# Attention and two dense layers on one core: order of the attention output copy, of the first dense slot, of the last keys' bank and of one store

## The reference

```python
# 1. attention, batch 4, 8 heads, 576 positions, head dimension 64
scores = (1/sqrt(64)) * q @ k.T + bias          # bias: a small net of |i-j| and i, per head
attn = exp(scores - rowmax) / (rowsum + 1e-9)
x = concat_heads(attn @ v)                      # 2304 tokens x 512
# 2. first dense layer, 512 -> 2048 -> 512
h = x @ w_in
y = (h - tanh(h)) @ w_out
# 3. second dense layer, 512 -> 1536 -> 512
g = y @ w_gate
out = (g * sigmoid(g) * (y @ w_val)) @ w_out2
```

## Time and profile before

| | us |
|---|---|
| median of 3 runs | 1259.72 |
| lowest and highest of them | 1258.40, 1260.73 |
| the profiled execution, its own time | 1260.17 |
| its span, first to last instruction | 1258.4 |
| PE busy | 1182.5 (94%) |
| DVE, ACT, POOL busy | 606.4, 574.2, 520.7 |
| bias table | to about 75 |
| plain heads and edge slot | about 75 to 138 |
| unit 0 with its eight large slots | 138 to 259 |
| units 1 and 2, large slots | 259 to 491 |
| units 3 and 4, short slots | 491 to 728 |
| rest of the first layer, second dense layer | to the end |

### The profile page before, as it was taken

How to read it: one execution, slowest core, us unless ns; L and a number is a source line. 1 busy time by engine, 2 the same in 40 slices (tenths; PEclk the granted TensorE clock), 3 DMA queues, 4 the chain that set the end, 5 groups by cost and what they waited for, 6 DMA issues and landing times.

```text
span 1258.4 us, 20260 instructions
## 1 busy us (share of the span) xinstructions
PE 1182.5 (94%) x7320; PEld 1082.7 (86%) x7320; DVE 606.4 (48%) x1377; ACT 574.2 (46%) x1163; POOL 520.7 (41%) x584
## 2 busy tenths in 40 slices
PE   5778799999999998999999999999999999999998
PEld 2345588889888988999899999999999999999998
DVE  8966677665566555666666643521211212112111
ACT  6977566655555555555555554521212222122212
POOL 2036577655555554877777722111111111111111
PEclk9999899999999999999999999999999999999999
DMA  5887464343434332544445343300000000000000
GB/s 172 260 264 222 129 190 143 110 128 104 115 108 128 110 99 81 156 133 139 138 142 137 111 157 126 126 26 1 27 26 26 26 22 30 1 26 1 26 1 26
DMA packets 80067, 125.46 MB, mean 100 GB/s; under 512 B 19424, under 2 KB 42976, under 8 KB 79968
## 3 DMA queue, kind: packets, MB, share of 16 engines
q1 hardware_dynamic: 79968, 124.17, 32.9%
HBM read 104.07 MB, written 20.05 MB: 99 GB/s over the span
## 4 chain that ended last, share of the span: by engine, by line
PE 76%; DVE 11%; issue 5%; ACT 5%; DMA 1%; SPq 1%; DVEq 0%; ACTq 0%
PE ps_s L1535 12%; PE ps_y L1546 12%; PE ps_h L1423 11%; PE ps_y L1442 11%; PE ps_h L1535 6%; PE ps_pt L1535 6%; PE ps_s L1343 5%; PE ps_pt L1362 5%; PE ps_pt L1396 3%; DVE feat L1058 3%; DVE prob L1091 2%; DVE g_b L1124 1%; PE ps_pt L1423 1%; ACT tanh_b L810 1%; DVE xy_stage L1132 1%
## 5 line engine op out<-in xcount | busy, mean ns | idle before, releaser
L723 POOL TENSOR_TENSOR fr<-tanh_b,fr 128x384 fp32r<-128x384 f32 x72 | 73.1, 1016 | 378.0 <-ACT fr L988 378.0
L1442 PE MATMUL ps_y<-fr,wbuf 128*128 128x384 f32 x1152 | 225.7, 336 | 0.0
L666 POOL TENSOR_SCALAR prob<-prob,rowinv 128x576 f32<-128x576 f32 (+1 forms) x160 | 122.4, 765 | 210.8 <-DVE rowinv L1102 195.0
L1423 PE MATMUL ps_h<-fr,wbuf 128*128 128x384 f32 x1056 | 206.6, 340 | 0.5 <-DVE g_b L1124 0.4
L1442 PEld LDWEIGHTS ps_y<-fr,wbuf 128*128 128x128 f32 x1152 | 198.9, 188 | 0.0
L1423 PEld LDWEIGHTS ps_h<-fr,wbuf 128*128 128x128 f32 x1056 | 181.9, 189 | 1.4 <-DVE g_b L1124 0.9
L785 ACT ACTIVATE prob<-prob,negmax 128x576 f32<-128x576 f32 (+1 forms) x160 | 124.0, 775 | 119.1 <-DVE negmax L1091 118.6
L1546 PE MATMUL ps_y<-wbuf,fr 128*128 128x512 f32 x648 | 161.1, 393 | 0.0
L671 POOL TENSOR_TENSOR fr<-g_b,fr 128x384 fp32r<-128x384 f32 x96 | 96.7, 1007 | 126.5 <-ACT fr L816 126.4
L1546 PEld LDWEIGHTS ps_y<-wbuf,fr 128*128 128x128 f32 x648 | 120.5, 188 | 22.1
L1362 PE MATMUL ps_pt<-ident,prob 128*128 128x128 f32 (+1 forms) x640 | 87.7, 264 | 40.4 <-DVE xy_stage L1132 26.3
(11 more groups left out here) (128 smaller groups left out, 1952.5 us busy)
## 6 DMA issues: line engine op xcount, KB each, us to landing
biasb<-bias_scratch SPq DMA_DIRECT2D x128, 216.0 KB, 2.7
raw<-k_t SPq DMA_DIRECT2D x59, 288.0 KB, 3.0
bias_scratch<-w_raw SPq DMA_DIRECT2D x72, 144.0 KB, 3.2
biasb<-bias_scratch SPq DMA_DIRECT2D x64, 144.0 KB, 2.9
w_raw<-w_chunks SPq DMA_DIRECT2D x16, 512.0 KB, 5.6
prob<-w_chunks SPq DMA_DIRECT2D x8, 768.0 KB, 4.2
raw<-v_p SPq DMA_DIRECT2D x32, 160.0 KB, 2.3
biasb<-bias_scratch SPq DMA_DIRECT2D x64, 72.0 KB, 2.6
```

Source lines behind the costliest of these rows:

```text
L666: eng.tensor_scalar(row, row, rowinv[0:hd.rows, tile % PR:tile % PR + 1], 1.0, ALU.mult, ALU.mult).then_inc(p_norm, 1)
L1423: mm = eng.matmul(hidden_bank(u, c)[:, 0:TOK], w[:, cols], x[:, d, :], start=d == 0 and i == 0, stop=d == KC - 1 and i == 2)
L1442: mm = eng.matmul(ps_y[:, d, 0:TOK], w[:, cols], g[c % 2], start=c == 0 and i == 0, stop=c == C1 - 1 and i == 2)
```

## The change

- **Large slots.** On ACT `o_part` of head v comes ahead of `tanh` of the slot's second chunk and its `g_high`; on DVE `x_out` comes ahead of that chunk's `gated`. It was the other way round.
- **First dense slot** (unit 0, chunks 0 and 1). `tanh` and `gated` of chunk 0 are the first work of ACT and DVE; PE's `gaps` become `[4, 2, 0]`, so chunk 1's hidden pieces come after tile 0 and two model pieces after tile 1. `inverse` of tile 1 of head 8 moves into the edge slot. In the edge slot ACT computes both exponentials before `o_part`, and DVE scores both tiles before `x_out`.
- **Last keys of plain heads** go to bank `ps_h` (tile 1's) instead of `ps_pt` (tile 0's). The wait for their copy moves from tile 0's transposes to tile 1's, the transposes of the last keys wait for tile 1's copy, and DVE's `pt_copy_end` moves ahead of `inverse` of tile 1. The first hidden piece of all waits for that bank too.
- **Short slots.** In a unit's last slot ACT's `x_high` comes before `o_part`, and DVE's `x_low` of the last quarter comes after `inverse`.
- **SP** issues the first quarter of `store_y` before the load of q instead of after it; in units with large heads the load of q comes later anyway, so nothing changes there.

```diff
@@ SP, loop over heads
                 following = HEADS[n + 2:n + 3]
+                if hd.unit > 1 and n == FIRST_OF[hd.unit] + 1:
+                    store_y(hd.unit - 2, 0)
                 for nxt in following:
                     if not ended(hd):
                         load_q(nxt)
                 for t in range(hd.nt):
-                    if t == 0 and hd.unit > 1 and n == FIRST_OF[hd.unit] + 1:
-                        store_y(hd.unit - 2, 0)
@@ ACT, edge
                 o_part(HEADS[v.n - 1], moe)
                 exp_tile(q, 0)
+                exp_tile(q, 1)
                 o_part(v, moe)
                 q_high(p, moe)
-                exp_tile(q, 1)
@@ ACT, short
                 g_high(u, c)
+                if late(moe):
+                    x_high(u + 1)
                 o_part(v, moe)
                 if q is not None:
                     exp_tile(q, 1)
-                if late(moe):
-                    x_high(u + 1)
@@ ACT, slot
+                if v.n == H:
+                    tanh(*moe[0])
                 pt_high(v, 0, moe)
...
                 exp_tile(q, 0)
-                if not first:
+                if not first and v.n > H:
                     tanh(*moe[0])
...
                 for t in range(2, q.nt):
                     exp_tile(q, t)
+                o_part(v, moe)
                 tanh(*moe[1])
                 g_high(*moe[1])
-                o_part(v, moe)
@@ DVE, pt_copy_end
-                eng.tensor_copy(plain_end(hd), ps_pt[64:P, 0:TOK]).then_inc(v_pt, 1)
+                eng.tensor_copy(plain_end(hd), ps_h[64:P, 0:TOK]).then_inc(v_pt, 1)
@@ DVE, alone
+                    if t == q.nt - 1 and v is not None:
+                        pt_copy_end(v)
                     if t > 0:
                         inverse(q, t - 1)
-                if v is not None:
-                    pt_copy_end(v)
@@ DVE, edge
                 score(q, 0, moe)
+                score(q, 1, moe)
+                inverse(q, 0)
                 x_out(v, moe)
                 x_high_last(0)
                 x_low(0, 1)
-                inverse(q, 0)
-                score(q, 1, moe)
+                inverse(q, 1)
+                score(q, 2, moe)
                 q_low(p, moe)
-                score(q, 2, moe)
@@ DVE, short
                     x_high_last(u + 1)
-                    x_low(u + 1, 1)
                 if q is not None:
                     inverse(q, 1)
                 if late(moe):
+                    x_low(u + 1, 1)
                     x_low(u + 1, 0)
@@ DVE, slot
+                if v.n == H:
+                    gated(*moe[0])
                 pt_low(v, 0, moe)
                 if v.n == H:
-                    inverse(v, 1)
                     inverse(v, 2)
...
-                if not first:
+                if not first and v.n > H:
                     gated(*moe[0])
...
+                x_out(v, moe)
                 gated(*moe[1])
-                x_out(v, moe)
@@ PE, transposed (plain heads)
-                    if t == 0:
+                    if t == 1:
                         eng.wait_ge(v_pt, splits(last, 0) + 1)
@@ PE, transposed_end
-                    eng.wait_ge(a_pt, copies(hd, 0) + 1)
+                    eng.wait_ge(a_pt, copies(hd, 1) + 1)
                 for t in range(hd.nt):
-                    mm = eng.transpose(ps_pt[:, tile_cols(hd, t)], prob[:, (hd.tile0 + t) % PR, S - P:S], ident[:, :])
+                    mm = eng.transpose((ps_pt if moe else ps_h)[:, tile_cols(hd, t)], prob[:, (hd.tile0 + t) % PR, S - P:S], ident[:, :])
@@ PE, hidden_pieces
+                        if (u, c) == (0, 0):
+                            eng.wait_ge(v_pt, splits(HEADS[H], 0))
@@ PE, slot
                 if moe[0] == (0, 0):
                     layer_work(4)
-                    gaps = [0, 0, 2]
+                    gaps = [4, 2, 0]
```

## The result

| | before | changed |
|---|---|---|
| median, us | 1260.09 (4 runs, 1258.40 to 1260.73) | 1241.99 (4 runs, 1241.34 to 1242.51) |
| the profiled execution, its span | 1260.17, 1258.4 | 1242.15, 1240.3 |
| PE busy | 1182.5 | 1179.8 |

The ratio is 0.9858, with a 95% interval of 0.9841 to 0.9875: the changed kernel is faster by 1.4%, 18.1 us. I had said 1248.5 (1242 to 1255); the median lies at the lower end of that range. So the direction is right and the size is a third too small.

The account below looks back on a forecast made before the run. PE sets the pace in units 1 and 2, stopping once per slot for `x_out`; ACT and DVE bound about half of unit 0's slots. Terms -12.6+2.6+2.1+1.5-1.6-3.3 = -11.3 us gave 1248.5 (1242 to 1255).

Parts of the forecast that it names:

- rival 1: Unit 0 and the first slot cost nothing: POOL idle for `w1_low`, first slot's order pays for itself; 1242.2, chance 0.16.
- Units 1 and 2: Inner slot ends: `x_out` ends at E+1.15 (E: attention output's last matmul's end), PE no longer waits; 1.05 each, 12.6 in all.
- what I gave back: Inner slots of units 1 and 2: 0.15 each, since ACT's copy of tile 0 starts at E+2.30, not E+2.05.
- almost no slack: Units 1 and 2: the chain from ACT's copy of tile 0 feeds the last keys' transposes so tightly that 0.15 is lost.
- Entries of units 1 and 2: `pt_low` of tile 0 comes at E+5.3 instead of E+6.07: -0.8 each, -1.6 together.
- Unit 0: Slots after the first: ACT and DVE's chain delays the `w1_low` pair; +0.33 for six slots, +0.57 for the seventh, +2.6.
- Rival 2: VectorE and GpSimd alternate at every slot end of unit 0: +7.7 instead of +2.6; 1253.5, chance 0.16.
- First dense slot: PE idles 3.5 before two model pieces waiting for `split_g`: +2.1, plus one clock drop, +1.5.
- Units 3 and 4: Entries: earlier y store ends `o_part`'s wait; -2.3 at unit 4, -1.0 at unit 3, -3.3 together.
- if it takes no longer than now: Entries of units 3 and 4: the y store, issued at 616.95, lands before 620.5, at its old duration (2.8 at unit 3).
- Plain heads: The 7.1 us wait for the last keys' copy moves by one tile, its end stays: 0.
- Rivals 3 and 4: 3: ACT's chain bounds units 1 and 2, 1258.5, chance 0.05; 4: clock stays low in unit 0, 1271.5, chance 0.04.

Follow-up runs that it names:

- e5_y_store_old: The changed kernel with the first quarter of the y store issued behind the load of q again; 1243.5 us, ratio 0.9870.
- e7_copy_between: The changed kernel with large slots' output copy between tanh and the high part on ACT, and DVE's output addition after the subtraction of tanh; 1234.2 us, ratio 0.9801.
- e4_bank_old: The changed kernel with the last keys of plain heads in the old bank and DVE's copy of them behind the inversion again; 1241.1 us, ratio 0.9853.
- e6_w1_between: The changed kernel with ACT's two weight copies at unit 0's slot ends between tanh and the gated chunk's high part; 1230.5 us, ratio 0.9769.

## Why the prediction was right, and where its sizes were off

The direction and the larger mechanisms were right. The number owes something to chance: the profile has -18.0 for the -11.3 of the sum, of which -1.96 is scatter of the start. The other 4.8 are units 1 and 2 (-2.2), unit 0 (-2.0), the entries of units 1 and 2 (-1.2), the first slot (-0.7), unit 3 (+1.3), unit 4 (-0.1) and the rest (+0.15). The measured 1242.0 is also what rival 1 had (1242.2), but not for its reasons: unit 0 does cost next to nothing (+0.63), yet the first slot's new order costs 2.89, and the sum comes out there since units 1 and 2 gave more.

**Units 1 and 2.** Right mechanism, 1.23 per slot for 1.05. `x_out` came at E+1.2 and PE's three pieces covered it. The term that was too small is what I gave back: ACT's copy of tile 0 does start late (341.34, behind `g_high`), but the slots are 13.22 long, so the chain behind it still meets the last keys' transposes, and nothing of the 1.20 bound was lost. The step that failed is "almost no slack". The kernel with that edit alone shows this.

**Entries of units 1 and 2.** -1.4 each for -0.8. The missed part is that DVE's instructions run shorter when they no longer meet POOL. The long `x_low` ahead of the earlier trace rows took 2.00 in the kernel before, where POOL had begun a step of v's split (L658) at 260.04:

```profile
260.31 2.00 DVE fr L1141
```

In the changed kernel it starts ahead of POOL's next `norm`:

```profile
260.19 1.08 POOL L671 TENSOR_TENSOR fr<-g_b,fr 128x384 fp32r<-128x384 f32 x1 [3.46 <-ACT fr L816]
...
261.20 1.36 DVE L1143 TENSOR_TENSOR fr<-xy_stage,fr 128x1152 fp32r<-128x1152 f32 x1 [0.79 <-ACT fr L830]
261.25 1.93 POOL L666 TENSOR_SCALAR prob<-prob,rowinv 128x576 f32<-128x576 f32 x1
```

Here DVE takes 1.36 and POOL's `norm`, 0.75 elsewhere, takes 1.93: it waited instead, and ends 0.62 behind `x_low`. The Trainium skill's rule ("SBUF — State Buffer", "Who interferes with whom"), that whoever issues first has the port for a whole instruction, agrees with both cases.

**Unit 0.** Right that PE's gain is worth nothing there and that the slots get slightly longer: +0.09 each on average, where I had +0.37. Before, slots of 14.48 and 14.94 took turns; now all are 14.73 to 14.81. So the short ones, which PE had bounded, grew by 0.3, and the long ones, whose chain I had forecast to grow by 0.11, shrank by 0.15. `pt_low` comes at E+4.35 (188.37-184.02), not E+4.68: the weight copies start at E+2.10 rather than E+2.30, and the pair starts at E+2.74 beside `split_g`, where I had let it wait for its end. Rival 2, the alternation at every slot end, is refuted: POOL waited, and DVE did its pair in one go, in 1.69. Rival 1 is near the measured length of the stage, but its reason fails: the pair takes 1.29 where POOL is idle, and not here. That this chain is the bound was the step worth most: moving two copies by a microsecond brought 9.7 us.

**First dense slot.** Right in mechanism and nearly in size (+2.9 for +3.6). The old order takes 15.20, and with the new one it takes 17.16 or 17.18 in two kernels in which the clock stayed at 2.4 GHz, +2.0 for +2.1. PE stood for 3.2 before the model pieces, for 3.5. Where the clock fell the slot took 18.09 (here), 17.84 and 18.53, so the clock's part was +0.9 here and +0.7 to +1.4 in all, for the +1.5 I took.

**Units 3 and 4.** Unit 4 -2.4 for -2.3. At unit 3 the step that failed is that the store lands early enough "if it takes no longer than now": it took 4.5, where it had taken 2.8, and `o_part` still waited for it for 1.54 (0.38 at unit 4). The +0.29 of this one trace is its worst case, though. Four more traces have the same code at that entry and took 25.26, 26.12, 26.21 and 26.24, against 26.91 before: -1.65 where the store came in time, -0.7 to -0.8 where it came late, for the forecast -1.0. Only the changed kernel's own trace had the clock fall there. I also missed a wait: in a unit's first slot the model pieces of the unit before follow right behind tile 0's scores and need `split_g`, which the new order delays.

```profile
476.98 2.35 PE L1448 MATMUL ps_y<-fr,wbuf 128*128 128x384 f32 x12 [1.03 <-POOL fr L671]
```

I had named `split_g` for inner slots only. At the entries of units 1 and 2 PE waits for it too (0.94 at 261.32), but its next transposes, at 263.52, stand behind `x_low` and `pt_low`. The clock fell at 485.8, half a microsecond after PE's idle 1.78 had ended with the transposes at 485.26: the scores and hidden pieces of the slot behind it run at the half clock there.

**Plain heads.** Right: the wait moved to tile 1, and a steady slot lasts 6.57 for 6.54. The -1.96 of the profile is scatter of the start.

**Rivals 3 and 4** did not come: no slot of unit 1 was longer than 13.25, and the clock was back within 4 us after each drop of the changed kernel.

## What to carry to other kernels

List what an engine's order puts between the event that frees a shared bank and the instruction that gives it back, and price each slot class by who sets its pace: the same edit gave 1.2 us per slot where PE was the bound and cost 0.1 where ACT and DVE were. A step moved off one such path is queued behind something else, so look for its users in the rare slots as well: the first slot of a unit had another order and another user. Where an engine other than PE sets the pace, fill its idle gaps with work that a second engine waits for: in unit 0 that brought 9.7 us, where the change had cost 0.6.

## What the runs showed of the hardware

- An instruction's length on DVE or POOL depends on which of them came first. A pair of `w1_low` took 1.29 with POOL idle and 1.69 beside it; a `norm` of 0.75 took 1.70 or 1.93 when DVE was at work. An edit that moves either changes lengths that the profile of before shows as fixed.
- How long a small store takes is not fixed by its place in the queue. Issued 0.4 us behind the load of v, its waiter started 2.5 us after the issue at unit 4 and 4.5 at unit 3 of the same execution; in e5_y_store_old, behind the load of q, it was 2.7 at unit 3.
- After the same idle time of 3.20 the clock stayed at full speed in two kernels (e5_y_store_old, e7_copy_between) and fell in three. In e4_bank_old it fell at 144.4, just ahead of the six matmuls behind the wait, which took 2.29; in the changed kernel at 147.8, 1.0 after they began, and they took 1.50; in e6_w1_between at 147.2, as they ended, and they took 1.31. The slot was 18.53, 18.09 and 17.84 long in that order. This is the changed kernel's fall and its return within 4 us (columns as in the earlier trace rows):

```profile
146.80:148.00 1.20, 1.16 (x6) 1.16 (x7) 0.00 (x0) 0.00 (x0) 0.71 (x1) 0.94 0.79 202
148.00:150.00 2.00, 2.00 (x10) 1.71 (x8) 0.14 (x1) 0.60 (x1) 0.00 (x0) 0.50 0.60 175
150.00:152.00 2.00, 1.55 (x9) 1.40 (x9) 1.16 (x2) 1.01 (x2) 1.58 (x2) 0.69 0.02 7
152.00:156.00 4.00, 2.65 (x15) 2.03 (x15) 2.62 (x7) 1.85 (x4) 0.70 (x1) 1.00 0.35 85
```
